# Hash-bucket attention with two MoE layers: q, k and the hash projection laid out on the host instead of on the chip

## The reference

```python
batch, n_heads, seq, head_dim = (2, 8, 768, 64)      # q, k, v; proj is (64, 6)
q_bits = (np.einsum('bhsd,dk->bhsk', q, proj) > 0)
k_bits = (np.einsum('bhsd,dk->bhsk', k, proj) > 0)
q_bucket = np.sum(q_bits * powers, axis=-1)
k_bucket = np.sum(k_bits * powers, axis=-1)
mask = q_bucket[:, :, :, None] == k_bucket[:, :, None, :]
scores = scale * np.matmul(q, k.transpose(0, 1, 3, 2))
scores = np.where(mask, scores, -1000000000.0)
attn = np.exp(scores - np.max(scores, axis=-1, keepdims=True))
attn = attn / (np.sum(attn, axis=-1, keepdims=True) + 1e-09)
attn_out = np.matmul(attn, v)
# x = attn_out as (1536, 512)
# MoE: argmax over 8 experts, out = gate * (relu(x @ w1[e]) @ w2[e])
# FFN: h = x @ w_in; g = max(h, 0) + alpha * min(h, 0); g @ w_out
```

## Time and profile before

| | |
|---|---|
| median of 3 runs | 693.76 us |
| the profiled execution | 693.38 us |
| its span | 691.5 us (1.9 us lie around it) |
| TensorE busy | 685.2 us, 99% |
| VectorE, ScalarE, Pool busy | 462.9, 356.9, 225.2 us |
| granted TensorE clock | 1.00 in every slice |

### The profile page before, as it was taken

How to read it: one execution, slowest core, us unless ns; L and a number is a source line. 1 busy time by engine, 2 the same in 40 slices (tenths; PEclk the granted TensorE clock), 3 DMA queues, 4 the chain that set the end, 5 groups by cost and what they waited for, 6 DMA issues and landing times.

```text
span 691.5 us, 12374 instructions
## 1 busy us (share of the span) xinstructions
PE 685.2 (99%) x4064; PEld 611.6 (88%) x4066; DVE 462.9 (67%) x996; ACT 356.9 (52%) x724; POOL 225.2 (33%) x325
## 2 busy tenths in 40 slices
PE   8999999999999999999999999999999999999998
PEld 5899999999999989989988998888888888888886
DVE  6988988889899989513411216666676666666664
ACT  6888888888888793224311215333343333433332
POOL 8855465555657961412014200500017000010000
PEclk9999999999999999999999999999999999999999
DMA  7985766748363510791114008200003000010001
GB/s 186 210 251 172 200 206 154 222 116 251 97 162 98 196 42 24 255 342 59 45 61 106 17 31 274 61 0 0 0 17 106 0 0 0 1 62 0 0 0 61
DMA packets 48243, 70.58 MB, mean 102 GB/s; under 512 B 7294, under 2 KB 27470, under 8 KB 48198
## 3 DMA queue, kind: packets, MB, share of 16 engines
q1 hardware_dynamic: 42036, 57.60, 29.2%
q0 software_dynamic: 2832, 8.45, 4.2%
q10 hardware_dynamic: 3330, 3.97, 1.6%
HBM read 33.46 MB, written 17.30 MB: 73 GB/s over the span
## 4 chain that ended last, share of the span: by engine, by line
PE 93%; DVE 3%; ACT 2%; DMA 1%; issue 1%; ACTq 0%; DVEq 0%
PE bank L1017 8%; PE bank L1246 6%; PE bank L1247 6%; PE bank L1248 6%; PE bank L1258 6%; PE bank L1259 6%; PE bank L1260 6%; PE bank L1036 4%; PE bank L1001 4%; PE bank L1038 4%; PE bank L1002 4%; PE bank L1187 3%; PE bank L1189 3%; PE bank L1191 3%; PE bank L1151 3%; PE bank L1150 3%
## 5 line engine op out<-in xcount | busy, mean ns | idle before, releaser
L1361 ACT ACTIVATE probs<-bank,raffine 128x768 f32<-128x768 f32 x96 | 95.2, 992 | 26.5 <-DVE raffine L1658 26.3
L1650 DVE TENSOR_REDUCE bank<-bank 128x1 f32<-128x768 f32 x96 | 92.2, 960 | 5.8 <-PE bank L1002 4.9
L1017 PE MATMUL bank<-cst,probs 128*128 128x128 f32 x576 | 80.5, 274 | 1.1 <-DVE pt_lo L1666 0.6
L1515 ACT ACTIVATE wi_hi<-ff_raw 128x512 fp32r (+1 forms) x48 | 30.4, 633 | 91.5 <-PE bank L1248 89.3
L1936 DVE SCALAR_TENSOR_TENSOR ht_lo<-bank,ht_hi 128x512 fp32r<-128x512 f32 x28 | 19.0, 689 | 85.2 <-ACT ht_hi L1457 85.2
L1666 DVE TENSOR_TENSOR pt_lo<-bank,pt_hi 128x384 fp32r<-128x384 f32 x128 | 70.5, 551 | 7.9 <-ACT pt_hi L1378 7.1
L1017 PEld LDWEIGHTS bank<-cst,probs 128*128 128x128 f32 x576 | 67.3, 141 | 8.9 <-issue 3.5
L1246 PE MATMUL bank<-x_hi,wi_hi 128*128 128x512 f32 (+1 forms) x192 | 74.4, 387 | 0.0
L1247 PE MATMUL bank<-x_lo,wi_hi 128*128 128x512 f32 (+1 forms) x192 | 73.9, 385 | 0.0
L1248 PE MATMUL bank<-x_hi,wi_lo 128*128 128x512 f32 (+1 forms) x192 | 73.9, 385 | 0.0
L1036 PE MATMUL bank<-pt_hi,v_split 128*128 128x384 f32 x192 | 72.6, 378 | 0.0
(11 more groups left out here) (329 smaller groups left out, 1631.9 us busy)
## 6 DMA issues: line engine op xcount, KB each, us to landing
stacks<-nat SPq DMA_DIRECT2D x84, 192.0 KB, 4.4
y_slots<-zeros SPq DMA_DIRECT2D x14, 512.0 KB, 5.3
w_raw<-in_moe_w SPq DMA_DIRECT2D x6, 1024.0 KB, 9.9
ff_raw<-in_moe_w_in SPq DMA_DIRECT2D x8, 512.0 KB, 6.4
ff_raw<-in_moe_w_out SPq DMA_DIRECT2D x4, 1024.0 KB, 9.2
y_slots<-y_sb ACTq DMA_DIRECT2D x14, 256.0 KB
v_raw<-in_v SPq DMA_DIRECT2D x16, 192.0 KB, 3.7
x_rows<-x_out SPq DMA_DIRECT2D x8, 384.0 KB, 3.0
```

The costliest lines, as they stand in the source:

```text
L1017: mm = pe.transpose(lane[1 + hf][:, t * P:t * P + P], probs[:, m % 3, kt * P:kt * P + P], C["ident"])
L1361: act.activation(probs[:, m % 3, :].rearrange("p (a c) -> p a c", a=2), s_ps[m % 2], ACT.Exp, bias=raffine[:, col, 1:2], scale=raffine[:, ...
L1650: dve.tensor_reduce(rmin_ps[n % 2], s_ps[n % 2], AX.XY, ALU.min).then_inc(rmin_done, 1)
```

## The change

The host now hands over q and k as [pair, head and head_dim (128), 768 columns], in the order in which the transposes gave them, and the projection as a [128, 2, 128] array that already holds its copies and zeros. Raw data land by DMA in `q_even`, `q_odd`, `k_even`, `k_odd` (SBUF, two buffers for each of q and k). TensorE's `turn_raw` and Pool's `pair_up` are gone. ScalarE's `high` and VectorE's `low` read SBUF in place of PSUM. The low part of k moves from VectorE to Pool (`k_lows`) for pairs 1 to 7; for pair 1 it stands ahead of Pool's four DMA issues and casts. In `feats` TensorE starts when the high part is there and waits for the low part before its third product. At the start one DMA of 128 KB brings the projection (3 KB before), ScalarE and VectorE make the two w tensors with one instruction each, and TensorE runs 9 filler products where it ran 14, and 3 fewer after the first transposes.

```diff
-WARM = (14, 12, 9, 3, 3)
+WARM = (9, 12, 9, 3)
 ...
-                sp.dma_start(q_raw[:].rearrange("p a t d -> p a (t d)"), q_pairs[pair]).then_inc(q_in, 16)
+                    sp.wait_ge(q_lo_done, split_no(1, pair - 2))
+                sp.dma_start(raw("q", pair)[:], q[pair]).then_inc(q_in[pair % 2], 16)
 ...
-            def pair_up(kind, pair):
 ...
-                for hd in range(2):
-                    pool.tensor_copy(both[:, :, hd, :], raw[:, hd]).then_inc(paired, 1)
+            def k_lows(hf, pair):
+
+                cols = slice(hf * HALF, hf * HALF + HALF)
+                k_hi, k_lo = halves("k", pair)
+                pool.wait_ge(k_hi_done, split_no(hf, pair))
+                pool.tensor_tensor(k_lo[:, cols], raw("k", pair)[:, cols], k_hi[:, cols], ALU.subtract
+                                   ).then_inc(k_lo_done, 1)
 ...
-            pair_up("q", 1)
             copy_q(1)
             pool.wait_ge(q_copied, 4)
-            pair_up("k", 1)
             split_v(0)
+            for hf in range(2):
+                k_lows(hf, 1)
 ...
-                if s == 6 and j + 2 < PAIRS:
-                    pair_up("q", j + 2)
-                if s == 9 and j + 2 < PAIRS:
-                    pair_up("k", j + 2)
                 if 0 <= n - 2 < STEPS and on_pool(n - 2, 1):
                     turned(n - 2)
+                for kind, hf, pair in units_at(n) if n >= len(EARLY_UNITS) else ():
+                    if kind == "k":
+                        k_lows(hf, pair)
 ...
-            def turn_raw(kind, hf, pair, p_ps):
 ...
-                pe.wait_ge(qk_lo_done, turned_no(kind[1], hf, pair) + 1)
-                pe.matmul(p_ps, w[:], hi[:, cols], start=True, stop=False)
-                pe.matmul(p_ps, w[:], lo[:, cols], start=False, stop=False)
-                pe.matmul(p_ps, w2[:], hi[:, cols], start=False, stop=True).then_inc(feat_made, 1)
+                pe.wait_ge(made, split_no(hf, pair))
+                pe.matmul(p_ps, w_bits[:, side], hi[:, cols], start=True, stop=False)
+                pe.matmul(p_ps, w_bits2[:, side], hi[:, cols], start=False, stop=False)
+                pe.wait_ge(split, split_no(hf, pair))
+                pe.matmul(p_ps, w_bits[:, side], lo[:, cols], start=False, stop=True).then_inc(feat_made, 1)
 ...
-                    act.activation(q_hi[:, cols], p_ps, ACT.Copy, scale=-SCALE).then_inc(qk_hi_done, 1)
+                    act.activation(q_hi[:, cols], raw(kind, pair)[:, cols], ACT.Copy, scale=-SCALE
+                                   ).then_inc(q_hi_done, 1)
 ...
-                    dve.scalar_tensor_tensor(q_lo[:, cols], p_ps, -SCALE, q_hi[:, cols], ALU.mult, ALU.subtract
-                                             ).then_inc(qk_lo_done, 1)
+                    dve.scalar_tensor_tensor(q_lo[:, cols], raw("q", pair)[:, cols], -SCALE, q_hi[:, cols], ALU.mult,
+                                             ALU.subtract).then_inc(q_lo_done, 1)
```

More of the change, by code:

```diff
@@ L402, in build, with raw, split_no @@
         comb4 = comb[:].rearrange("p (g a) c -> p g a c", a=2)
[L404 to L411, removed]
+        def raw(kind, pair):
+            return ((q_even, q_odd) if kind == "q" else (k_even, k_odd))[pair % 2]
+        def split_no(hf, pair):
+            return 2 * pair + hf + 1
         def feat_no(kind, hf, pair):
@@ L448, in stack_q @@
                 par = pair % 2
-                sp.wait_ge(qk_lo_done, turned_no("q", 1, pair) + 1)
+                sp.wait_ge(q_lo_done, split_no(1, pair))
                 if pair >= 2:
@@ L465, in stack_k @@
                 par = pair % 2
-                sp.wait_ge(qk_lo_done, turned_no("k", 1, pair) + 1)
+                sp.wait_ge(k_lo_done, split_no(1, pair))
                 if pair >= 2:
@@ L966, in make_unit @@
                     fold(at, p_ps)
-                elif kind in ("q", "k"):
-                    turn_raw(kind, at, pair, p_ps)
                 elif kind == "rows":
@@ L1072, in _ @@
                     first_up(1, (0, 1))
-                for at, unit in enumerate(units_at(n)):
-                    wait_unit(held[at])
-                    held[at] = unit
+                for unit in units_at(n):
+                    if unit[0] in ("q", "k"):
+                        continue
+                    wait_unit(held)
+                    held = unit
                     for no, made in enumerate((COUNT_STEP, RANK_STEP, INDEX_STEP)):
@@ L1095, in _ @@
                         mm.then_inc(index0_made, 1)
-                    make_unit(unit, place(at))
+                    make_unit(unit, lane[0])
             def route_counts():
@@ L1332, in split_rows, with high @@
                                ACT.Copy).then_inc(bx_hi, 1)
-            def high(unit, p_ps):
+            def high(unit):
                 kind, hf, pair = unit
@@ L1418, in _ @@
             move_feats("fk", 0, fk_moved)
-            high(("q", 1, 0), first_bank("q", 1))
+            high(("q", 1, 0))
             shift_q(1)
@@ L1432, in _ @@
                     turned(n - 2, 1)
-                for at, unit in enumerate(units_at(n)):
-                    high(unit, place(at))
+                for unit in units_at(n):
+                    high(unit)
                 for fc in PIECES.get(n, ()):
@@ L1605, in _ @@
             dve.memset(credit[:, 4:5], 0.0).then_inc(idx_set, 1)
[L1606 to L1612 removed]
+            dve.wait_ge(shift_zeroed, 1)
+            dve.wait_ge(w_made, 1)
+            dve.tensor_tensor(w_bits2[:], proj_raw[:], w_bits[:], ALU.subtract).then_inc(sel_ready, 1)
             def split_rows(i, tt, src):
@@ L1618, in split_rows, with low @@
                                   xt_hi[:, :, tt * P:tt * P + P], ALU.subtract).then_inc(bx_lo, 1)
-            def low(unit, p_ps):
+            def low(unit):
                 kind, at, pair = unit
@@ L1811, in step @@
                 else:
-                    for at, unit in enumerate(units):
-                        low(unit, place(at))
+                    for unit in units:
+                        low(unit)
                 if 56 <= n < STEPS + 2:
@@ L1828, in _ @@
             for kind, hf in (("k", 0), ("k", 1), ("q", 0)):
-                low((kind, hf, 0), first_bank(kind, hf))
+                low((kind, hf, 0))
+            dve.wait_ge(cst_in, 16)
             for hf in range(2):
@@ L1832, in _ @@
             first_features("fq", 0, BOT, 0, fq_first)
-            low(("q", 1, 0), first_bank("q", 1))
+            low(("q", 1, 0))
             for n in range(STEPS + QT):
@@ L2155, with laid_out @@
         "moe2_w_in", "moe2_w_out", "moe2_alpha"]
+def laid_out(name, a):
+    if name in ("q", "k"):
+        a = a.reshape(PAIRS, 2, P, QT, HD).transpose(0, 1, 4, 3, 2).reshape(PAIRS, P, SEQ)
+    if name == "proj":
+        both = np.zeros((P, 2, P), a.dtype)
+        for rows, at in ((slice(0, HD), HD), (slice(HD, P), 0)):
+            for side, apart in ((0, 2 * BITS), (1, BITS)):
+                for col in (at, at + apart):
+                    both[rows, side, col:col + BITS] = a
+        a = both
+    return np.ascontiguousarray(a)
 def kernel(**inputs):
@@ L2164 @@
     for name in _INS:
-        a = np.ascontiguousarray(inputs[name])
+        a = laid_out(name, inputs[name])
         if a.dtype.kind in "iu":
```

117 lines of the change are left out of this document (40 added, 77 removed).

## The result

The changed kernel takes 696.26 us (median of 7 runs, 694.61 to 697.64) where the kernel before, beside it, takes 693.75 (693.40 to 693.78): ratio 1.0036, interval 1.0027 to 1.0046. It is slower by 2.5 us; 691.1 was forecast, with a range of 687.4 to 694.0. The profiled execution took 696.09 us, span 694.2, mean granted clock 0.995. Its lines are renumbered: scores L973 and L974, `turn_probs` L990, `values` L1007 and L1009, `feats` L888 to L891, low part of q L1595, Pool's `k_lows` L663, its halves L683 and L685.

The account below looks back on a forecast made before the run. It took TensorE as the bound, with a loop through VectorE and ScalarE close under it. Start +1.7 and steady steps -4.3 gave -2.6 us: 690.8 from the profiled 693.38, 691.1 as median, range 687.4 to 694.0.

Parts of the forecast that it names:

- The first scores come 1.5 us sooner: Start: Pool's copies begin at 6.25, so first scores come at 9.5 us instead of 11.01; bounds 0.7 and 2.4.
- rival 4: Steady `q` threes: VectorE's low parts and Pool exclude each other, 5.4 us in all, 696.5 us; chance 0.12.
- TensorE is 1.7 us later: Step 6: `values(1)` waits 3.2 us for Pool's queue, ending 1.7 us later than before.
- The queue itself: Pool after the two `k_lows`: 9.44 us of work without a pause, TensorE waiting 3.2 us for it.
- the forecast 16.6: Step 2: ScalarE's first high part of k of pair 1 done at 16.6 us, letting `k_lows` start.
- 7.14 for every three: Every three steps with `q` or `k` units take 7.14 us instead of 7.50; 12 threes gain 4.3 us.
- Threes with `fq` and `fk` unchanged: Three-step groups with `fq` and `fk` units keep their length.
- 4.3 was forecast: Steady steps: 12 x (7.50 - 7.14) = 4.3 us gained, bounds 2.0 and 7.9.
- Rival 1: Start: Pool's queue doesn't hold TensorE, -1.5 - 4.3 = -5.8, 687.9 us; chance 0.17.
- Rivals 2 (6.84): Steady threes: TensorE's whole time comes back and Pool doesn't hold it, -1.5 - 7.9, 684.4 us; chance 0.05.
- 3 (7.33): Steady threes: `high` from SBUF delays exponentials, threes stay at 7.33, 693.4 us; chance 0.21.

Follow-up runs that it names:

- Experiment two: Changed kernel with Pool's first copy waiting for VectorE's low part of the first half of q: 694.89 us, ratio 1.0019.
- experiment four: Changed kernel with 14 filler matmuls in step 6 just ahead of the values of step 1: 694.03 us, ratio 1.0001.
- experiment seven: Kernel with both Pool edits (690.47 us), leaving out most of VectorE's second-half low part in every third step: 686.66 us, ratio 0.9903.
- experiment one: Changed kernel with Pool's two `k_lows` of pair 1 moved behind its DMA issues and casts: 691.43 us, ratio 0.9963.
- the warm start: Kernel with both Pool edits (690.47 us), with 11 filler matmuls instead of 3 ahead of the first scores: 690.07 us, ratio 0.9950.

## Why the prediction was wrong

*"The first scores come 1.5 us sooner": failed.* The step took Pool's chain alone and began it rightly, but left VectorE's low part of q at 0.55 us, beside Pool's copies. The prediction had the mechanism, and rival 4, and priced it only in the steady steps. It acted at the start: 3.03 us. Experiment two shows it, with 0.9 us of the 1.5; the other 0.6 is the order itself (Pool 0.25 us later) and the same collision at the second low part of q. A small slip beside it: from Pool's last copy to the first scores the sum took 0.17 us, have 11.01 - 10.80 = 0.21; it changes nothing.

*"TensorE is 1.7 us later": right in mechanism, mis-sized.* The queue itself was right (9.41 us for 9.44, a wait of 3.05 us for 3.2). But step 9 came 5.2 us later. The start that didn't come (1.5 us) and a first three at half clock (0.6) moved ScalarE's high parts and so `k_lows` from the forecast 16.6 to 18.81, 2.2 us; `values(1)` from 28.0 to 30.28. The matmuls at 1.2 GHz after the wait put 1.3 us on top (experiment four). 1.7 + 2.3 + 1.3 = 5.3, against 5.2. The sum had no term for the clock, since every slice of before stood at 1.00: a wait that a change adds has no clock in the rows of before.

*"7.14 for every three": right within 0.06 for nine of twelve.* Four `q` threes take 7.08, `k` threes 7.19 (four), 7.08 (at 72) and 7.36 (at 60, 7.71 before). These ten gained 3.58 us, 0.36 each on average, as forecast, though one value was given for what turned out to be several: 0.40 for `q`, 0.30 for most `k`. The cause given, VectorE's second low part, is shown for `q` by experiment seven and not for four of the `k` threes. The two threes at 57 and 69 lost 0.63 us instead of gaining 0.72.

*"Threes with `fq` and `fk` unchanged": nearly.* They got longer by 0.05 us each, 0.37 over all twelve (the one at 75 got shorter by 0.22). In all 2.95 - 0.37 = 2.6 us came back where 4.3 was forecast.

*Rivals.* Rival 4 came nearest in time (696.5) and wrong in place: no steady low part of q is held (mean 0.55 in all 14). Its mechanism costs 0.9 us at the first scores (1.6 at step 3, with the clock) and, at 57 and 69, 0.63 + 0.72 = 1.4. Rival 1's condition, a queue that doesn't hold TensorE, is what experiment one makes; 3.5 us of its 5.8 were missing then, in the start and at 57 and 69. Rivals 2 (6.84) and 3 (7.33) fell: nine of the twelve threes take 7.08 to 7.19.

## What to carry to other kernels

When an input moves from PSUM to SBUF on VectorE, walk through every place where that instruction stands, the start too, and write beside it what Pool runs there and what waits for it; the neighbours behind it count as well. Before work is put ahead of others in an engine's queue, ask when its input comes, not how long it runs: 2 us of `k_lows` cost 4.7. And to each new wait of TensorE belongs the price of the clock after it.

## What was not expected of the hardware

- A VectorE instruction that begins 0.08 us ahead of Pool's first copy was still held, through four Pool copies in a row (3.03 us for 0.55), where 0.25 us ahead of Pool's subtraction it was not (0.58). By the rule of the Trainium skill on issue order ("SBUF — State Buffer", section "Who interferes with whom") VectorE should have gone first at 6.13; the recorded starts there say otherwise. Nor did a change from one Pool copy to the next let it in.
- One wait of 3.05 us took the clock from 2.4 to 1.2 GHz for about 2.7 us of products; cost 1.3 us.
- A cast of 128x6 elements with a single SBUF input was held behind Pool's subtraction (0.98 us for 0.22), like the 128x48 subtraction with two (1.02 for 0.26).
- The executions of the changed kernel spread over 3.0 us (694.61 to 697.64), those of before beside them over 0.4 (in a later comparison over 2.0, 693.04 to 695.09), and with the warm start over 0.1 (689.99 to 690.10). That the clock falls in one execution and not in another is seen in the six traces of one start (granted clock from 5 to 20 us between 0.77 and 1.00); that it makes the whole spread is only likely.
- Moving two small instructions by one step changed the order of VectorE and Pool 12 steps later, and gave back 0.9 of the 1.5 us there (0.4 of it came in again at 84 and 90).
